# Attention step with one transpose group ahead of its first scores, the output behind the fifth group and evictions dealt anew, with 64-token expert blocks

## The reference

```python
# q, k, v: (4, 8, 1152, 64)
q_pool = q.reshape(B, H, S // 2, 2, D).mean(axis=3)            # 576 queries a head
scores = scale * np.matmul(q_pool, k.transpose(0, 1, 3, 2))    # 576 x 1152
attn = np.exp(scores - np.max(scores, axis=-1, keepdims=True))
attn = attn / (np.sum(attn, axis=-1, keepdims=True) + 1e-09)
x = np.matmul(attn, v)                                         # heads side by side: (4, 576, 512)
# experts: e = argmax(x @ w_gate), or the expert of the token before
# where sigmoid(x @ w_local) >= 0.5
out[b, s] = p[e] * (np.maximum(x[b, s] @ w1[e], 0.0) @ w2[e])
```

## Time and profile before

| | |
|---|---|
| median of 3 runs | 920.35 us (919.35 to 921.61) |
| the profiled execution | 920.67 us, its span 918.8 us |
| busy share of the span | PE 93%, PEld 59%, DVE 51%, ACT 43%, POOL 36% |
| TensorE clock granted, mean | 0.963 of 2.4 GHz |
| attention, about | 0 to 551 us |
| routing and experts, about | 553 to 919 us |

### The profile page before, as it was taken

The page is one execution under the profiler, slowest core; times in us unless marked ns, Lnnn a source line. Parts: engine busy times, 40 slices in busy tenths (PEclk is TensorE's granted clock), DMA queues, the critical chain, the costliest instruction groups (busy, mean ns, idle before and its releaser), DMA issues. The chain is left out here.

```text
span 918.8 us, 14574 instructions
## 1 busy us (share of the span) xinstructions
PE 855.1 (93%) x5478; PEld 541.0 (59%) x5479; DVE 471.9 (51%) x628; ACT 399.1 (43%) x567; POOL 330.1 (36%) x322
## 2 busy tenths in 40 slices
PE   5899999999999999999999992889999999999995
PEld 4677787777777788777777762533333333333331
DVE  4797575666657656566665646323232323232321
ACT  1555555655655555465564530233323232323230
POOL 7572474365357347436535000112121222222211
PEclk6899999999999999999999995799999999999997
DMA  9523524443352443444331009664333840100000
GB/s 218 144 58 96 133 70 108 108 111 89 91 136 59 106 122 76 109 101 114 85 91 34 10 11 343 237 205 148 103 130 122 262 164 34 34 30 29 27 30 18
DMA packets 48799, 96.40 MB, mean 105 GB/s; under 512 B 23727, under 2 KB 23727, under 8 KB 48752
## 3 DMA queue, kind: packets, MB, share of 16 engines
q1 hardware_dynamic: 45472, 85.51, 33.4%
q0 software_dynamic: 3280, 10.23, 3.3%
HBM read 86.28 MB, written 9.96 MB: 105 GB/s over the span
## 5 line engine op out<-in xcount | busy, mean ns | idle before, releaser
L627 DVE TENSOR_REDUCE negmax<-psum 128x1 f32<-128x1152 f32 x144 | 195.3, 1357 | 109.5 <-PE psum L388 93.1
L388 PE MATMUL psum<-kstack,qstack 128*128 128x384 f32 x768 | 171.7, 360 | 10.3 <-DVE kstack L300 6.4
L527 ACT ACTIVATE probs<-psum,negmax 128x1152 f32<-128x1152 f32 x128 | 156.3, 1221 | 49.5 <-DVE negmax L627 45.7
L413 PE MATMUL psum<-ident,probs 128*128 128x128 f32 x1152 | 160.6, 275 | 18.0 <-DVE x_out L661 13.9
L413 PEld LDWEIGHTS psum<-ident,probs 128*128 128x128 f32 x1152 | 134.5, 142 | 31.1 <-DVE x_out L661 21.3
L962 PE MATMUL psum<-wbuf,xgT 128*64 x320 | 145.2, 608 | 3.9 <-ACT second L900 2.7
L981 PE MATMUL psum<-wbuf,shared 128*64 x320 | 144.2, 604 | 3.8 <-DVE second L1151 3.8
L388 PEld LDWEIGHTS psum<-kstack,qstack 128*128 128x128 f32 x768 | 132.3, 194 | 25.2 <-issue 12.4
L522 ACT ACTIVATE pT<-psum 128x512 f32<-128x512 f32 x160 | 95.2, 595 | 117.9 <-PE psum L413 117.9
L964 PE MATMUL psum<-second,xgT 128*64 128x512 f32 x320 | 145.2, 607 | 0.0
L983 PE MATMUL psum<-second,shared 128*64 128x512 f32 x320 | 144.2, 604 | 0.0
(11 more groups left out here) (174 smaller groups left out, 947.7 us busy)
## 6 DMA issues: line engine op xcount, KB each, us to landing
wbuf<-in_w SPq DMA_DIRECT2D x64, 512.0 KB, 5.0
qraw<-in_q_t SPq DMA_DIRECT2D x64, 288.0 KB, 5.0
kraw<-in_k_t SPq DMA_DIRECT2D x64, 288.0 KB, 6.1
vraw<-in_v_t SPq DMA_DIRECT2D x16, 576.0 KB, 4.9
x_rows<-x_out SPq DMA_DIRECT2D x32, 128.0 KB, 2.0
x_rows<-x_out SPq DMA_DIRECT2D x32, 16.0 KB, 1.8
xg<-x_rows,src_now POOLq DMA_INDIRECT x21, 3.5
out<-shared,dst_now POOLq DMA_INDIRECT x20, 4.0
```

The costliest lines, as they stand in the source:

```text
L388: last = nc.tensor.matmul(dst[:, third, 0:THIRD], qstack[p % 2][:, part, tile_cols(side, i)], kstack[p % 2][:, side, third * THIRD:(third ...
L413: last = nc.tensor.transpose(dst[:, i * P:(i + 1) * P], probs[side][:, i, c * P:(c + 1) * P], ident[:])
L527: nc.scalar.activation(probs[side][:, i, :].rearrange("p (a b) -> p a b", a=3), slot(f, i)[:, :, 0:THIRD], ACT.Exp, bias=negmax[:, p % 2, ...
L627: nc.vector.tensor_reduce(negmax[:, p % 2, col:col + 1], slot(f, i)[:, :, 0:THIRD], AX.XY, ALU.max, negate=True).then_inc(max_ready, 1)
```

## The change

On PE, T0 goes ahead of S0, and each later transpose group moves one place forward: T1 and T2 behind S0, T3 and T4 behind S1, and T5 alone stands behind the output. `OUT_AFTER` becomes 4, so the bank numbers run T0 T1 T2 T3 T4 output T5 T6 and so on. T5 then waits for the eviction of T4, and T6 for DVE's scaling of the output. ACT evicts T0, T1, T3, T6 and T8 (before: 0, 2, 4, 6, 8), DVE T2, T4, T5 and T7 (before: 1, 3, 5, 7). The identity part of `project` is built ahead of the first keys, the gate part at the end of step 1, and the three routing functions move to the ends of steps 3, 5 and 7. The expert stage is not touched.

```diff
-OUT_AFTER = 3
+OUT_AFTER = 4
...
@@ block.tensor @@
         for f in PHASES:
+            if weighed(f):
+                turn(f, 0)
             if scored(f):
                 score(f, 0)
             if weighed(f):
-                turn(f, 0)
                 turn(f, 1)
+                turn(f, 2)
             if scored(f):
                 score(f, 1)
             if weighed(f):
-                turn(f, 2)
                 turn(f, 3)
+                turn(f, 4)
             if scored(f):
                 score(f, 2)
             if projected(f):
                 output(f)
             if weighed(f):
-                turn(f, 4)
                 turn(f, 5)
...
@@ block.scalar @@
             if weighed(f):
                 save_t(f, 0)
+                save_t(f, 1)
             if scored(f):
                 take_exp(f, 0)
             if weighed(f):
-                save_t(f, 2)
+                save_t(f, 3)
             if scored(f):
                 take_exp(f, 1)
-            if weighed(f):
-                save_t(f, 4)
-            if scored(f):
                 take_exp(f, 2)
...
-        def projection():
+        def projection_identity():
+            for half in range(2):
+                rows = slice(half * DH, (half + 1) * DH)
+                nc.vector.tensor_copy(project[rows, :, 0:DH], ident[rows, rows].unsqueeze(1).broadcast_to([DH, HEADS, DH]))
+
+        def projection_gates():
             dve.wait_ge(gates_loaded, 32)
             for half in range(2):
                 rows = slice(half * DH, (half + 1) * DH)
-                nc.vector.tensor_copy(project[rows, :, 0:DH], ident[rows, rows].unsqueeze(1).broadcast_to([DH, HEADS, DH]))
                 nc.vector.tensor_copy(project[rows, :, DH:OCOLS], gates_raw[rows]).then_inc(project_ready, 1)
...
+        projection_identity()
         for side in range(2):
             dve.wait_ge(k_loaded[side], 32)
...
@@ block.vector @@
             if weighed(f):
-                save_t(f, 1)
+                save_t(f, 2)
             if scored(f):
                 take_max(f, 1)
             if weighed(f):
-                save_t(f, 3)
+                save_t(f, 4)
...
-            if f == 0:
-                projection()
             if f == 1:
+                projection_gates()
+            if f == 3:
                 routing_constants_a()
-            if f == 2:
+            if f == 5:
                 routing_constants_b()
-            if f == 3:
+            if f == 7:
                 routing_constants_c()
```

## The result

The changed kernel took 894.02 us (median of 4 runs, 891.5 to 896.55) against 920.31 us, a ratio of 0.9719 (95% interval 0.9693 to 0.9745). A second set of runs gave 896.43 us (5 runs, 894.55 to 900.06) and 0.9751 (0.9732 to 0.9771). The forecast was 899.3, with a range of 896.5 to 905. It was in the right direction and about four fifths of the size.

The account below looks back on a forecast made before the run. The prediction took PE to set the pace, with its waits for other engines as the loss. Steady steps 19.7 plus weigh-tail wait 1.4 made 21.1 us off 920.67, less 0.3 for the median: 899.3, range 896.5 to 905.

Parts of the forecast that it names:

- the covers: Steady steps: time to spare before PE would wait, 0.40 for T6 and 0.17 for the weigh group.
- S2's wait: Steps 2 to 31: S2's waits for an exponential, 7.2 us in all, were to stay.
- The weigh-tail wait of step 2: Step 2: PE's wait for DVE's save of the weigh tail was to go, saving 1.4 us.
- the stall per step: T5's wait for DVE's scaling of the output: 0.73 per even, 0.58 per odd step, 19.7 us saved in all.
- the start: Up to step 2: taken as 0 us saved, range -0.5 to +1.
- the expert stage: Routing and experts: as long as before, difference 0.
- the layout of step 1: Step 1 with T0 ahead of S0, at half clock first: step 2 at about 43.2 us, 0.5 saved.
- Part of the gain coming back at DVE's evictions: Rival: in steady steps the weigh group waits for late DVE evictions, time 904 to 908; chance 0.12.
- the wait moving to T6: Rival: in steady steps T6 takes over the whole stall, time 919 to 921; chance 0.03.
- T0 waiting for ACT: Rival: a late ACT eviction of the weigh group holds T0 and S0 back, time 932; chance 0.04.
- The rule on DVE and GpSimd: End of step 1: DVE's two-port copies and GpSimd exclude each other, so moved gate copies are short; 0 in the sum.
- The rule on the clock: Start: transposes don't count alike as clock activity, so T0 ahead wouldn't raise the clock; some 0.6 us later, 899.9.

Follow-up runs that it names:

- moves_only: The kernel before with only the copies for project and the routing constants moved, order and bank numbers as before: 911.75 us.
- order_only: The changed kernel with the copies for project and the routing constants put back at their old places: 898.08 us.
- expert_fill: The changed kernel with 40 in place of 24 identity transposes ahead of the experts; expert stage 361.76 us, whole time not given.
- tail_late: The changed kernel with each even step's weigh tail moved behind S0 of the next odd step; 31.31 us per two steps, whole time not given.
- after_again: The changed kernel once more, unchanged: 896.43 us, ratio 0.9751 to the kernel before.
- step1_before: The changed kernel with step 1 alone in the old order and old deal of evictions: ratio 0.9722 to the kernel before.
- bank_only: The kernel before with T4 moved ahead of the output and OUT_AFTER 4, T0 still behind S0; steps 2 to 31 took 473.01 us.
- bank_moves: bank_only with the copies for project and the routing constants moved as in the change: 894.35 us.
- start_fill: The changed kernel with 14 more identity transposes on PE behind S3 of step 0; step 2 started at 41.58 us, whole time not given.
- deal_before: The changed kernel's PE order and bank numbers, with evictions dealt to ACT and DVE as before: 922.30 us.

## Why the prediction was wrong

**The mechanism was right.** The stall before T5 came from the bank numbers, it went in all 30 steps, nothing took its place, and the covers were as worked out (0.40 forecast for T6 and 0.34 found, 0.17 forecast and found for the weigh group). S2's wait stayed. The weigh-tail wait of step 2 went, 1.35 to 1.6 us by moves_only and order_only against a forecast of 1.4. Three terms of the sum were mis-sized: the stall per step, by 2.1 us in all, the start, by 1.3, and the expert stage, by 1.5, for which the range had nothing.

**The stall per step.** The step "a transpose group on its own takes 0.41" took T5's length behind a wait. Without the wait S3 follows T5 by 0.35 (205.43 to 205.78). The even step shrank by 0.81 (16.35 to 15.54), not 0.73, and the odd one by 0.63 (16.40 to 15.77), not 0.58. In all, steps 2 to 31 lost 23.2 against 21.1; 15 of each and the weigh tail's 1.35 make 22.95, and 0.2 stays open. The weight loads' own 21.0 in the earlier trace rows with the 1.4 would have given 22.4, nearer the truth; the text named it and took the lower number.

**The start.** The forecast was 0, with -0.5 to +1, and it was -1.3. The step that failed is not the layout of step 1 but what was made of it. The layout gave 0.5 saved, with S2 at 32.3, S3 at 34.4, the tail round at 36.5 and step 2 at 43.2, and the forecast took 0. expert_fill, with the same code in step 1, has 32.38, 34.54, 36.49 and 43.23. There T0 and S0 ran at half clock, as laid out:

```profile
25.86 1.12 PE L413 MATMUL psum<-ident,probs 128*128 128x128 f32 x4 [2.79 <-ACT probs L528]
26.63 2.27 PE L388 MATMUL psum<-kstack,qstack 128*128 128x384 f32 x6
```

In the changed kernel the clock was still up as T0 began (the us from 25.00 has a granted clock of 1.00 there, and 0.50 in tail_late), T0 took 0.81, S1 ran at full clock (1.29 for 1.49 in expert_fill), and step 2 came at 42.39, at 42.49 in after_again. So the other 0.8 us are the clock's state in these executions, which the bounds left out.

The layout also hid that two large effects meet here. Moving the copies alone saves 4.5 us (moves_only), T0 ahead alone 0.2 (order_only), and both together 1.3: once the copies are gone, T0 ahead costs 2.8 to 3.7 (against step1_before), and with them in place nothing. That S0 ran at full clock in moves_only may be chance: in bank_only, with the copies at their old place, S0 at 24.04 took 1.32 too, and in bank_moves, with them moved, 2.29.

**The expert stage.** "The expert stage as long as before" was right in the mean and wrong as a bound. Its length was 359.5 to 364.5 us over 13 profiles of kernels with the same expert code (the last two with other warm-up). One difference can be seen. PE waits once near 600 us before and 575 after, and has lost its full clock behind it or not:

```profile
600.00:604.00 4.00, 3.23 (x10) 1.10 (x12) 0.00 (x0) 0.96 (x2) 0.00 (x0) 0.71 0.86 302
604.00:608.00 4.00, 4.00 (x18) 1.29 (x16) 0.00 (x0) 0.60 (x1) 0.00 (x0) 0.87 0.65 220
```

These are windows of the kernel before, with the granted clock third from the right, 0.71 and 0.87. The changed kernel at the same place:

```profile
576.00:580.00 4.00, 2.62 (x12) 0.95 (x14) 0.00 (x0) 1.57 (x2) 0.00 (x0) 1.00 0.84 308
580.00:584.00 4.00, 4.00 (x22) 1.34 (x18) 0.00 (x0) 0.60 (x1) 0.00 (x0) 1.00 0.84 263
```

From the first transposes of h (L973) to the start of DVE's last copy of the second weights (L1151), the stage took 302.2 us in the five profiles that kept full clock there (the changed kernel, after_again, bank_only, bank_moves, start_fill) and 303.2 to 303.9 in the eight that had a dip to half clock, whichever kernel it was. From there on it was 17.0 to 18.2. The widest part is the one ahead, from routing to the first transposes of h: 39.2 to 43.4, the changed kernel 42.5 and before 41.4. The dips come and go with the same code, so the 1.5 us of the first comparison are chance, and the difference of 2.4 us between the two sets of runs of the same kernel is of that order. The range had no term for it. With 2 us more at either end, from that spread, a range of 894.5 to 907 would have followed from the same reasoning, and the measured 894.02 would still have been 0.5 outside, for the stall per step. Not settled is what decides whether the clock dips. Fuller work on PE ahead of the first tile (expert_fill) moved the dip and didn't remove it.

**The rivals.** Part of the gain coming back at DVE's evictions, the wait moving to T6 and T0 waiting for ACT did not happen. The rival that came nearest to harm was not among them: with the evictions left as they were, T0 ahead costs all that the bank numbers gain (deal_before).

**The rule on DVE and GpSimd.** The gate copies at the end of step 1 took 0.39 us for both, with POOL idle beside them, where one had taken 2.63 beside POOL's tensor_tensor:

```profile
39.73 0.39 DVE L624 COPY project<-gates_raw 64x72 f32<-64x72 f32 x2
```

The trace agrees with the Trainium skill's page "SBUF — State Buffer", section "Who interferes with whom", and the sum's 0 held.

**The rule on the clock.** The forecast told of the page "TensorE: Matmul & The Clock Gate", Part 4, of the Trainium skill, by which transposes don't count as the same activity. The runs speak against it. PE's first work in every kernel is 24 transposes of the identity (L482 from 1.52), with no matmul ahead of them. In the kernel before, windows of 1 us hold parts of 7 of them at first and of 11 later (the first bracket of each line):

```profile
2.52:3.52 1.00, 1.00 (x7) 1.00 (x6) 0.00 (x0) 0.00 (x0) 0.00 (x0) 1.00 0.89 258
4.52:5.52 1.00, 1.00 (x11) 0.94 (x9) 0.00 (x0) 0.00 (x0) 0.00 (x0) 1.00 1.05 221
```

The clock column is not to be read here, since the trace's first record of the clock, the full one, is at 4.3 us. So the clock rose behind transposes alone; all 24 took 4.18 us in this profile and 5.38 in tail_late's, where that record is at 6.9. In start_fill 14 transposes of the identity, with 12 score matmuls ahead of them, were followed by S0 at 1.31, and in the six profiles with T0 ahead and without them S0 took 2.23 to 2.27. That sign is weaker, since S0 also found full clock in bank_only and step1_before, with no such transposes.

## What to carry to other kernels

When two buffers turn in strict order among several producers, look at which eviction each wait really names, and give the number of a late one to a group with work ahead of it: here one number and the place of one transpose group (bank_only) gave 19.4 of the 23.2 us in the steady steps. Price a stall in an unchanging stretch by the weight loads' idle time or by a step that has no stall, not by a group that stands behind one. And where two edits act on the same short stretch, run each alone and both together: here they gave 4.5 and 0.2 alone and 1.3 together, and such effects do not add. A start or a stage that no edit touches still needs a width in the range, taken from its length in several profiles; the same code reached step 2 at 42.39 to 43.29.

## What the runs showed of the hardware

- Where transposes follow the weigh group (64-wide weight loads) directly, the weight loads show up to 0.4 us of idle time: 6.2 us in 16 cases in the changed kernel, 11.1 in 29 with tail_late. On PE's starts it is 0.10: 0.53 us from the last matmuls of the weigh group to the transposes, 0.43 to the tail. Behind the tail, 64 wide too, there is none.
- Moving the tail's four groups to fill a wait of 0.24 cost as much as it filled: they added 1.37 us at the new place and 1.14 at the old.
- The clock rose from half to full while PE had done nothing but transposes of the identity (24 of them, in the kernel before the rise at 4.3 us).
- The same code had S0 of step 1 behind a T0 of 0.71 to 1.12 us, by whether the clock was still up as T0 began, and reached step 2 at 42.39 to 43.29.
